# Reordering the first microseconds of a sparse attention and two-layer MoE kernel

## The chip, the cores and the metric

The kernel runs on one core of a Trainium2 chip. The metric is the device time of one execution in microseconds; lower is better. The kernel before has a median of 600.24 us over 3 runs (599.21 to 602.61).

## The reference

The reference computes a blocked attention and passes its result through two feed-forward layers. All tensors are fp32.

```python
# attention: batch 2, 8 heads, 768 positions, head size 64; block 32, window 16
k_sum = k.reshape(B, H, nb, block, D).max(axis=3)
v_sum = v.reshape(B, H, nb, block, D).mean(axis=3)
scores_l = scale * q @ k^T      # kept where |i - j| < 16, else -1e9
scores_s = scale * q . k_sum + log(block)
a = exp(scores_all - max);  a = a / (sum(a) + 1e-9)
x = a @ concat(v, v_sum)        # -> (1536, 512)
# layer 1
h = max(x @ w_in, 0);  x = (h * h) @ w_out       # 512 -> 2048 -> 512
# layer 2: P, Q polynomials of h with coefficients a, b
out = (P(h) / (Q(h) + 1e-6)) @ w_out2
```

## The kernel before

The work has two parts. The attention stage handles 24 groups. A pair (two heads of one batch entry, `n`, 8 of them) has three groups `G`; a group is four windows of 64 queries. Behind it come layer 1 and layer 2, with every fp32 product made of three products of rounded halves on TensorE.

A group goes through the engines in this order. TensorE computes its scores (`scores(G)`, L465 against the keys, L474 against the block maxima) into PSUM. VectorE adds the mask and takes the row minimum (`masked`, L886). ScalarE takes the exponentials with their row sums (`exps`, L679). VectorE guards and inverts the sums (L893, L898). GpSimd multiplies by the inverse (`normalise`, L354). TensorE transposes (`turn`, L499), ScalarE copies the transposes out of PSUM (L706, tile `probT`), and TensorE multiplies with the values (`output`, L515). The value window of a pair (`vwin`) holds 96 rows loaded from memory and 24 rows of block means. For the means TensorE runs `summary(n)` (L485), ScalarE copies (`copy_sums`, L685), TensorE runs `gather(n)` (L492), ScalarE copies (`copy_summary`, L691), and GpSimd spreads them into the window (`spread`, L339). The block maxima of the keys are a reduction on VectorE (`block_max`, L871).

The order of the work on each engine is written out by hand, with one list per engine and semaphores between them. TensorE runs ahead: scores of groups 0 to 2 before the loop, group 3 and 4 in its first turn, and then four groups ahead. Before the first scores it multiplies zeros (`keep_busy`, L554), `WARM` times 512 columns.

All loads are issued by SP in program order, but for two of pair 0 that ScalarE issues at its start: the middle third of the keys and the first third of the queries (semaphore `q_first[0]`, for which scores of group 0 wait). SP issues the other two thirds of the keys, the rest of the queries, the value window of pair 0 in two halves of 288 KB, and then keys, queries and window of the next pairs, 384 + 384 + 576 KB each. From pair 3 on the keys wait for the scores of an earlier pair, since three buffers go round. ScalarE's stream begins with nine semaphore increments that give first credits; the two transfers stand behind them. On ScalarE the exponentials of groups 0, 1 and 2 come before the loop, with the copies of the means between, and turn `G` of the loop copies the transposes of group `G` and then takes the exponentials of group `G + 3`. On GpSimd the normalisations of groups 0 and 1 come first, and then the spread of group 0.

Of the kernel before, what the change touches and what calls it, by code (L numbers as in the profile page):

```python
# [28 lines left out]
P = 128  # L29
B, H, S, D = 2, 8, 768, 64  # L30
BLOCK, BAND = 32, 16
# [8 lines left out]
GROUPS = PAIRS * B * GPB  # L40
# [20 lines left out]
P_RING = 4  # L61
# [3 lines left out]
XPAIRS = GROUPS // 2  # L65
KP = S + 2 * BAND
THIRD = S // GPB
WARM = 3
SPLIT_AT = {9: 0, 10: 1, 12: 2, 13: 3, 15: 4, 16: 5}
SUMMARY_AT = [0] + [GPB * n - 2 - (n > 2) for n in range(1, NB)]  # L70

# [11 lines left out]
def build(nc, qT, kT, vw, w1, w2, coef_a, coef_b, out):  # L83
# [43 lines left out]
    q, kraw, vwin = [], [], []  # L127
# [44 lines left out]
    k_first = [sem(f"k_first{i}") for i in range(GPB)]  # L172
# [4 lines left out]
    q_first = [sem(f"q_first{i}") for i in range(2)]  # L177
# [25 lines left out]
    norm_done = sem("norm_done")  # L203
# [36 lines left out]
    @block.sync  # L240
    def _(sp):
        def load_k(n):
            if n >= RING:
                sp.wait_ge(s_done, GPB * (n - RING + 1) + 1)
            sp.dma_start(kraw[n % RING][:, BAND:BAND + S], kT[n]).then_inc(k_in[n % RING], 16)

        def load_k_first(i):
            sp.dma_start(kraw[0][:, BAND + THIRD * i:BAND + THIRD * (i + 1)],
                         kT[0][:, THIRD * i:THIRD * (i + 1)]).then_inc(k_first[i], 16)

        def load_q(n):
            if n >= RING:
                sp.wait_ge(s_done, GPB * (n - RING + 1) + 2)
            sp.dma_start(q[n % RING][:, :], qT[n]).then_inc(q_in[n % RING], 16)

        def load_vwin(n):
            if n >= 2:
                sp.wait_ge(s_done, GPB * (n - RING + 2) - (n == 2))
            if n >= V_RING:
                sp.wait_ge(o_done, done(2, GPB * (n - V_RING + 1) - 1))  # L260
            for half in (slice(0, NW // 2), slice(NW // 2, NW)):
                sp.dma_start(vwin[n % V_RING][0:KW, half, :], vw[n][:, half, :]).then_inc(vw_in[n % V_RING], 16)

        def load_first(j):
            sp.dma_start(wraw[:, j:j + 1, :], w1[j:j + 1].rearrange("a p n -> p a n")).then_inc(w_first[j], 16)

        def load_weights(w, j, index, turn):
            if not (isinstance(turn, int) and turn == 0):
                sp.wait_ge(w_in[index], 16 * turn)
            sp.dma_start(wraw[:, bass.ds(j, 1), :], w[bass.ds(j, 1)].rearrange("a p n -> p a n")).then_inc(w_in[index], 16)  # L270

        load_k_first(0)
        load_k_first(2)
        sp.dma_start(q[0][:, THIRD:], qT[0][:, THIRD:]).then_inc(q_first[1], 16)
        load_vwin(0)
        for n in range(1, NB):
            load_k(n)
            load_q(n)
            if n >= NB - 1 - EARLY and n < NB - 1:
                load_first(n - NB + 1 + EARLY)  # L280
            load_vwin(n)
        sp.dma_start(ca[:, :], coef_a.partition_broadcast(P)).then_inc(coef_in, 16)
        sp.dma_start(braw[:, :], coef_b.partition_broadcast(P)).then_inc(coef_in, 16)
        for j in range(EARLY, FT // 2):
            if j < EARLY + 3:
                sp.wait_ge(s_done, GROUPS - 2 + j - EARLY)
            else:
                sp.wait_ge(o_done, done(2, GROUPS - 7 + j - EARLY))
            load_weights(w1, j, *landing(j))
        sp.wait_ge(o_done, done(2, GROUPS - 1))  # L290
        with sp.Fori(0, FT // 2 // LAND) as k:
            for i in range(LAND):
                load_weights(w1, LAND * k + FT // 2 + i, *landing(FT // 2 + i, k))
        with sp.Fori(0, FT // LAND) as k:
            for i in range(LAND):

                sp.wait_ge(b_done, done(2, (NCH - 1) * FT + LAND * k + i))
                load_weights(w2, LAND * k + i, *landing(FT + i, k))
        rows = out.rearrange("(n p) d -> n p d", p=P)
        with sp.Fori(0, NCH) as c:  # L300
            for t in range(ROWS):
                sp.wait_ge(o_copied, done(ROWS, ROWS * c + t))
                sp.dma_start(rows[bass.ds(ROWS * c + t, 1)].rearrange("a p d -> p a d"),
                             osb[:, t:t + 1, :]).then_inc(out_written[t], 16)
        for t in range(ROWS):
            sp.wait_ge(out_written[t], 16 * (NCH + 1))
# [3 lines left out]
    def _(pool):  # L310
# [30 lines left out]
        def spread(G):  # L341

            n, gi = divmod(G, GPB)
            if gi == 0:
                pool.wait_ge(vsum_copied, n + 1)
                if n >= V_RING:
                    pool.wait_ge(o_done, done(2, GPB * (n - V_RING + 1) - 1))
            pool.wait_ge(norm_done, min(G + 2, GROUPS))
            copy(vwin[n % V_RING][KW:COLS, GU * gi:GU * (gi + 1), :],
                 vsum[n % 2][KW:COLS, :].unsqueeze(1).to_broadcast([NBLK, GU, P])).then_inc(spread_done, 1)  # L350

        def normalise(G, r):
            pool.wait_ge(inv_done, G + 1)
            g.tensor_tensor(prob[r][:, :, :], prob[r][:, :, :],  # L354
                            inverse[r][:, :].unsqueeze(2).to_broadcast([P, GU, COLS]), ALU.mult).then_inc(norm_done, 1)
# [7 lines left out]
            pool.wait_ge(sem_hi, n + 1)  # L363
            g.tensor_tensor(wlo[index], wraw[index], whi[index].bitcast(F32), ALU.subtract).then_inc(sem_lo, 1)

        for G in range(2):
            normalise(G, G)
        spread(0)
        pool.wait_ge(spread_done, 1)

        def split_in(x):

# [64 lines left out]
    def _(pe):  # L437
# [5 lines left out]
        def scores(G):  # L443

            n, gi = divmod(G, GPB)
            r = n % RING
            if n == 0 and gi < 2:
                pe.wait_ge(q_first[gi], 16)
            if gi == 0:
                if n > 0:  # L450
                    pe.wait_ge(q_in[r], 16 * (n // RING + (r > 0)))
                if n == 0:
                    pe.wait_ge(edges, 1)
                    for part in range(GPB):
                        pe.wait_ge(k_first[part], 16)
                else:
                    pe.wait_ge(k_in[r], 16 * (n // RING + (r > 0)))
            pe.wait_ge(s_free, done(2, G - 2))

            for j in range(GU // 2):  # L460
                for e in range(2):
                    w = GU * gi + 2 * j + e
                    for h in range(2):
                        rows = slice(D * h, D * h + D)
                        mm(sps[G % 2][h][QW * e:QW * e + QW, j * COLS:j * COLS + KW], q[r][rows, QW * w:QW * w + QW],  # L465
                           kraw[r][rows, QW * w:QW * w + KW], start=True, stop=True)
            if gi == 0:
                pe.wait_ge(ksum_done, GPB * (n + 1))
            for j in range(GU // 2):
                for e in range(2):  # L470
                    w = GU * gi + 2 * j + e
                    for h in range(2):
                        rows = slice(D * h, D * h + D)
                        last = mm(sps[G % 2][h][QW * e:QW * e + QW, j * COLS + KW:(j + 1) * COLS],  # L474
                                  q[r][rows, QW * w:QW * w + QW], ksum[r][rows, :], start=True, stop=True)
            last.then_inc(s_done, 1)
# [82 lines left out]
        pe.wait_ge(consts, 4)  # L559
        scores(0)  # L560
        scores(1)
        pe.wait_ge(means_done, 1)
        summary(0)
        scores(2)
        pe.wait_ge(pick_ready, 4)
        keep_busy(2 * P)
        gather(0)
# [1 line left out]
        for G in range(GROUPS):  # L569
            turn(G, G % P_RING)  # L570
            ahead = 4 if G else 3
# [84 lines left out]
    @block.scalar  # L656
    def _(act):
        a = nc.scalar
        act.sem_inc(probT_done, 2)
        act.sem_inc(o_copied, ROWS)  # L660
        act.sem_inc(h_free, 2)
        act.sem_inc(y_free, KT)
        for t in range(ROWS):
            act.sem_inc(out_written[t], 16)

        act.dma_start(kraw[0][:, BAND + THIRD:BAND + 2 * THIRD], kT[0][:, THIRD:2 * THIRD]).then_inc(k_first[1], 16)
        act.dma_start(q[0][:, 0:THIRD], qT[0][:, 0:THIRD]).then_inc(q_first[0], 16)
        a.preload_act_table_set("natural_log_exp_and_others")
        act.wait_ge(consts, 3)
        act.wait_ge(means_clear, 1)  # L670
# [28 lines left out]
        copy_sums(0)  # L699
        exps(1, 1)  # L700
        copy_summary(0)
        exps(2, 2)
        for G in range(GROUPS):
            act.wait_ge(t_done, done(P_RING, G))
            act.wait_ge(o_done, done(2, G - 2))
            a.copy(probT[G % 2][:, :], tps[0:COLS, :]).then_inc(probT_done, 1)  # L706
            if G + 3 < GROUPS:
                exps(G + 3, (G + 3) % P_RING)
            if G == GROUPS - 2:
                relu(0, 0)  # L710
            for n in range(1, NB):
                if SUMMARY_AT[n] == G:
                    copy_sums(n)
                if SUMMARY_AT[n] + 1 == G:
                    copy_summary(n)
# [366 lines left out]
```

## Time and profile before

| | us |
|---|---|
| median of 3 runs | 600.24 |
| the profiled execution | 599.46 |
| its span in the profile | 597.6 |
| PE (TensorE) busy | 585.5 |
| DVE (VectorE) busy | 411.2 |
| ACT (ScalarE) busy | 290.0 |
| POOL (GpSimd) busy | 153.1 |

The span is what the profile's rows cover; the rest of the execution's time lies around it. PEld is TensorE's load of stationary operands, which overlaps its products. DVEq, ACTq and SPq are the instruction sequencers of the engines, which issue the transfers. The attention stage takes about the first 75 us.

### The profile page before, as it was taken

The page shows a single profiled execution, that of the slowest core. Times are in us where ns is not written, and L with a number is a line of the kernel's source. Part 1 is how long each engine was busy: PE and PEld are TensorE (multiplying, and loading weights), DVE is VectorE, ACT ScalarE, POOL GpSimd, SP SyncE. Part 2 cuts the span into 40 slices and gives each one's busy share as a digit, 9 for nine tenths or more (in the row PEclk, how much of TensorE's full clock was granted, in tenths as well). Part 3 has the DMA queues.
Part 4 walks back from the last instruction along what each step waited for, and adds up shares of the span by engine and source line. Part 5 has one row for each costly group of instructions (what it writes and reads, how often), then busy time and mean ns, then how long its engine had stood idle before and what let it go on. Part 6 is the DMA issues. An engine that isn't in the chain of part 4 may idle for free.

```text
span 597.6 us, 10616 instructions
## 1 busy us (share of the span) xinstructions
PE 585.5 (98%) x3770; PEld 479.4 (80%) x3770; DVE 411.2 (69%) x787; ACT 290.0 (49%) x613; POOL 153.1 (26%) x159
## 2 busy tenths in 40 slices
PE   7998999999999999999999999999999999999996
PEld 4777788888888888888888888888888888888884
DVE  5888796664433333456666788888888888888885
ACT  4888610111311101310111887777877767877775
POOL 4678810000120000300000355353242212231221
PEclk9999999999999999999999999999999999999999
DMA  8984570000000000032233200000100000100001
GB/s 254 261 242 109 168 281 1 0 1 0 2 0 0 0 0 0 0 107 83 94 105 106 70 1 1 0 0 1 71 0 0 0 0 0 71 0 1 0 1 70
DMA packets 11186, 31.42 MB, mean 53 GB/s; under 512 B 1552, under 2 KB 2064, under 8 KB 11152
## 3 DMA queue, kind: packets, MB, share of 16 engines
q1 hardware_dynamic: 10864, 30.68, 16.2%
q8 instruction: 24, 0.39, 0.3%
q10 hardware_dynamic: 288, 0.26, 0.1%
q14 instruction: 10, 0.08, 0.0%
HBM read 27.79 MB, written 3.15 MB: 52 GB/s over the span
## 4 chain that ended last, share of the span: by engine, by line
PE 50%; DVE 28%; issue 9%; ACT 7%; POOL 3%; DVEq 1%; ACTq 0%; POOLq 0%
PE bank L529 23%; PE bank L596 21%; DVE ratio L1024 6%; DVE numer L1006 6%; DVE ratio L1018 5%; DVE numer L1004 5%; DVE ratio L1013 5%; ACT hhi L764 5%; PE bank L515 2%; PE bank L499 1%; POOL prob L354 1%; ACT prob L679 1%; POOL vwin L339 1%; PE bank L465 1%; PE bank L554 1%
## 5 line engine op out<-in xcount | busy, mean ns | idle before, releaser
L529 PE MATMUL bank<-xhi,whi 128*128 (+1 forms) x384 | 149.9, 390 | 0.0
L529 PE MATMUL bank<-xhi,wlo 128*128 (+1 forms) x384 | 149.5, 389 | 0.0
L529 PE MATMUL bank<-xlo,whi 128*128 (+1 forms) x384 | 149.4, 389 | 0.0
L696 ACT ACTIVATE hsq<-bank 128x512 f32<-128x512 f32 x48 | 28.7, 598 | 213.3 <-PE bank L529 213.2
L407 POOL TENSOR_TENSOR denom<-denom,habs 128x512 f32<-128x512 f32 (+1 forms) x49 | 65.8, 1342 | 246.1 <-ACT denom L775 246.1
L529 PEld LDWEIGHTS bank<-xhi,whi 128*128 128x128 f32 x384 | 72.1, 188 | 15.0
L529 PEld LDWEIGHTS bank<-xhi,wlo 128*128 128x128 f32 x384 | 72.0, 188 | 15.0
L529 PEld LDWEIGHTS bank<-xlo,whi 128*128 128x128 f32 x384 | 72.1, 188 | 14.8
L613 PE MATMUL bank<-whi,hhi 128*128 128x512 f32 x192 | 74.8, 390 | 1.9 <-DVE hlo L1029 1.9
L1029 DVE TENSOR_TENSOR hlo<-ratio,hhi 128x512 fp32r<-128x512 f32 (+1 forms) x49 | 50.9, 1039 | 35.1 <-ACT hhi L764 35.1
L613 PE MATMUL bank<-wlo,hhi 128*128 128x512 f32 x192 | 74.7, 389 | 0.0
L613 PE MATMUL bank<-whi,hlo 128*128 128x512 f32 x192 | 74.7, 389 | 0.0
L596 PE MATMUL bank<-hhi,whi 128*128 128x512 f32 x192 | 74.7, 389 | 0.0
L596 PE MATMUL bank<-hlo,whi 128*128 128x512 f32 x192 | 74.7, 389 | 0.0
L596 PE MATMUL bank<-hhi,wlo 128*128 128x512 f32 x192 | 74.7, 389 | 0.0
L928 DVE TENSOR_TENSOR hsq<-hsq 128x512 f32<-128x512 f32 x48 | 34.0, 709 | 50.2 <-ACT hsq L696 50.2
L931 DVE TENSOR_SCALAR hhi<-hsq 128x512 fp32r<-128x512 f32 x48 | 21.4, 445 | 64.0 <-PE bank L596 63.8
L397 POOL TENSOR_TENSOR xlo<-xraw,xhi 128x512 fp32r<-128x512 f32 x12 | 19.2, 1624 | 165.1 <-ACT xraw L734 165.1
L772 ACT ACTIVATE habs<-bank 128x512 f32<-128x512 f32 x48 | 28.9, 602 | 52.7 <-PE bank L529 52.7
L613 PEld LDWEIGHTS bank<-whi,hhi 128*128 128x128 f32 x192 | 36.0, 188 | 10.0 <-issue 2.6
L613 PEld LDWEIGHTS bank<-whi,hlo 128*128 128x128 f32 x192 | 36.1, 188 | 7.6
L596 PEld LDWEIGHTS bank<-hhi,wlo 128*128 128x128 f32 x192 | 36.1, 188 | 7.5
(78 smaller groups left out, 890.5 us busy)
## 6 DMA issues: line engine op xcount, KB each, us to landing
wraw<-w SPq DMA_DIRECT2D x32, 512.0 KB, 3.4
vwin<-vw SPq DMA_DIRECT2D x16, 288.0 KB, 4.8
out<-osb SPq DMA_DIRECT2D x12, 256.0 KB, 2.1
kraw<-kT SPq DMA_DIRECT2D x7, 384.0 KB, 5.4
q<-qT SPq DMA_DIRECT2D x7, 384.0 KB, 4.5
kraw<-kT SPq DMA_DIRECT2D x2, 128.0 KB, 2.7
q<-qT SPq DMA_DIRECT2D x1, 256.0 KB, 4.6
kraw<-kT ACTq DMA_DIRECT2D x1, 128.0 KB, 3.3
```

Source lines behind the costliest of these rows:

```text
L407: g.tensor_tensor(denom[:, i, cols], denom[:, i, cols], habs[:, i, cols], ALU.mult).then_inc(q_done, 1)
L529: last = mm(hps[j % 2][:, :], W[a][:, j, kt * P:(kt + 1) * P], X[b][:, kt, bass.ds(CH * c, CH)], start=kt == 0 and i == 0, stop=kt == KT - ...
L596: last = mm(acc[dt][:, :], W[a][:, j, KT * P + dt * P:KT * P + (dt + 1) * P], HID[b][:, j % 2, :], start=j == 0 and i == 0, stop=j == FT - ...
L613: last = mm(acc[t][:, :], HID[a][:, j % 2, t * P:(t + 1) * P], W[b][:, j, KT * P:], start=j == 0 and i == 0, stop=j == FT - 1 and i == 2)
L764: a.copy(hhi[:, i, cols], ratio[:, cols]).then_inc(hi_done, 1)
L928: d.tensor_tensor(hsq[:, i, :], hsq[:, i, :], hsq[:, i, :], ALU.mult).then_inc(sq_done, 1)
L1004: d.tensor_tensor(numer[:, i, :], hps[i][:, :], numer[:, i, :], ALU.mult).then_inc(horner_done, 1)
L1006: d.scalar_tensor_tensor(numer[:, i, :], numer[:, i, :], ca[:, 1:2], hps[i][:, :], ALU.subtract, ALU.mult).then_inc(h_free, 1)
L1013: d.scalar_tensor_tensor(ratio[:, cols], denom[:, i, cols], one[:, 0:1], rcp0[bank][:, cols], ALU.add, ALU.mult).then_inc(t1_done, 1)
L1018: d.scalar_tensor_tensor(ratio[:, cols], ratio[:, cols], -2.0, rcp0[bank][:, cols], ALU.add, ALU.mult).then_inc(t2_done, 1)
L1024: d.scalar_tensor_tensor(ratio[:, cols], numer[:, i, cols], ca[:, 0:1], ratio[:, cols], ALU.subtract, ALU.mult).then_inc(ratio_done, 1)
L1029: d.tensor_tensor(hlo[:, i, cols], ratio[:, cols], hhi[:, i, cols].bitcast(F32), ALU.subtract).then_inc(g_ready, 1)
```

## The change

Seven edits, all in the first microseconds of the program:

```diff
-WARM = 3
+WARM = 2
@@ SP
         sp.dma_start(q[0][:, THIRD:], qT[0][:, THIRD:]).then_inc(q_first[1], 16)
+        sp.wait_ge(q_first[0], 16)
         load_vwin(0)
@@ GpSimd, in spread(G)
-            pool.wait_ge(norm_done, min(G + 2, GROUPS))
+            pool.wait_ge(norm_done, min(G + 2, GROUPS) if G else 1)
@@ GpSimd
-        for G in range(2):
-            normalise(G, G)
+        normalise(0, 0)
         spread(0)
         pool.wait_ge(spread_done, 1)
+        normalise(1, 1)
@@ TensorE
         scores(0)
         scores(1)
+        keep_busy(P)
+        scores(2)
         pe.wait_ge(means_done, 1)
         summary(0)
-        scores(2)
@@ ScalarE: the two dma_start move ahead of the nine sem_inc
+        act.dma_start(kraw[0][:, BAND + THIRD:BAND + 2 * THIRD], kT[0][:, THIRD:2 * THIRD]).then_inc(k_first[1], 16)
+        act.dma_start(q[0][:, 0:THIRD], qT[0][:, 0:THIRD]).then_inc(q_first[0], 16)
         act.sem_inc(probT_done, 2)
         ...
-        act.dma_start(kraw[0][:, BAND + THIRD:BAND + 2 * THIRD], kT[0][:, THIRD:2 * THIRD]).then_inc(k_first[1], 16)
-        act.dma_start(q[0][:, 0:THIRD], qT[0][:, 0:THIRD]).then_inc(q_first[0], 16)
@@ ScalarE
         exps(1, 1)
         copy_summary(0)
-        exps(2, 2)
         for G in range(GROUPS):
             act.wait_ge(t_done, done(P_RING, G))
             act.wait_ge(o_done, done(2, G - 2))
             a.copy(probT[G % 2][:, :], tps[0:COLS, :]).then_inc(probT_done, 1)
-            if G + 3 < GROUPS:
-                exps(G + 3, (G + 3) % P_RING)
+            for ahead in (2,) if G == 0 else (2, 3) if G == 1 else (3,):
+                if G + ahead < GROUPS:
+                    exps(G + ahead, (G + ahead) % P_RING)
```

With it, the copy of the first transposes precedes the exponentials of group 2, and the copy of the second transposes precedes those of group 3 and 4; from turn 2 on the order is as before. The spread of group 0 waits for normalisation 0 alone. SP issues the value window of pair 0, and all that follows, once the first third of the queries has landed.

## Rows read from the trace of the kernel before

**Rows 1.** The page's busy line, span and engines.
```profile
PE 585.5 (98%) x3770; PEld 479.4 (80%) x3770; DVE 411.2 (69%) x787; ACT 290.0 (49%) x613; POOL 153.1 (26%) x159
```

**Rows 2.** Stretches: from:to and length, then busy per engine, PEclk, DMA share, GB/s.
```profile
75.00:95.00 20.00, 20.00 (x89) 16.54 (x90) 18.38 (x27) 2.40 (x4) 2.12 (x2) 1.00 0.57 211
```

**Rows 3.** Chain that ended last, in order of time: start, duration, what.
```profile
1.81 4.59 PE bank L554 x6
...
6.64 0.54 PE bank L465 x14
...
13.83 0.59 ACT probT L706
...
14.47 0.69 PE bank L515 x16
...
32.99 0.05 ACT probT L706
...
38.16 0.99 POOL prob L354
...
57.75 0.63 POOL vwin L339
```

**Rows 4.** Line L554, two stretches: duration ns min/median/max, first to last start.
```profile
L554 PE MATMUL bank<-probT x2: 1007/1034/1061, 3.7 to 4.5; 120*128 120x512 f32 x2
...
L554 PE MATMUL bank<-probT x3: 592/593/1007, 4.5 to 5.8; 120*128 120x512 f32 x3
```

**Rows 5.** Timeline, the first issues of transfers: start, duration, engine, line.
```profile
0.82 0.87 SPq L248 DMA_DIRECT2D kraw<-kT  x2
1.35 0.39 ACTq L666 DMA_DIRECT2D kraw<-kT  x1
1.77 0.45 ACTq L667 DMA_DIRECT2D q<-qT  x1
2.21 0.90 SPq L262 DMA_DIRECT2D vwin<-vw  x2
```

**Rows 6.** Transfers issued at 1.77, 2.68 and 13.70: size, us to landing.
```profile
q<-qT ACTq DMA_DIRECT2D x1, 128.0 KB, 4.8
...
vwin<-vw SPq DMA_DIRECT2D x1, 288.0 KB, 5.8
...
kraw<-kT SPq DMA_DIRECT2D x1, 384.0 KB, 6.9
```

**Rows 7.** Stretches of 2 us; the last two columns are DMA share and GB/s.
```profile
2.00:4.00 2.00, 2.00 (x3) 0.97 (x4) 1.10 (x5) 1.66 (x4) 1.57 (x9) 1.00 0.81 225
4.00:6.00 2.00, 2.00 (x4) 0.55 (x3) 1.32 (x6) 0.00 (x0) 0.23 (x2) 1.00 1.11 332
6.00:8.00 2.00, 1.72 (x65) 1.25 (x64) 0.35 (x3) 0.00 (x0) 0.00 (x0) 1.00 0.97 237
...
18.00:20.00 2.00, 2.00 (x57) 1.70 (x54) 1.97 (x12) 1.95 (x10) 1.52 (x3) 1.00 1.06 288
```

**Rows 8.** Timeline of the front: start, duration, operation, [idle before <-releaser].
```profile
4.40 1.07 DVE L871 TENSOR_REDUCE ksum<-kraw 128x8 f32<-128x256 f32 x3
...
8.59 0.86 PE L485 MATMUL bank<-vwin,means 96*32 96x128 f32 x24 [0.62 <-issue]
...
10.11 0.24 ACT L685 COPY sums<-bank 128x128 f32<-128x128 f32 x1
...
13.54 0.62 POOL L339 TENSOR_SCALAR vwin<-vsum 24x512 f32<-24x512 f32 x1 [0.18 <-POOL prob L354]
```

**Rows 9.** Timeline of groups 4 to 6, 20 to 26 us.
```profile
20.62 0.42 DVE L871 TENSOR_REDUCE ksum<-kraw 128x8 f32<-128x256 f32 x1 [0.40 <-DMA kraw<-kT]
...
21.56 0.28 DVE L886 CUSTOM_DVE_ANT_0 prob<-bank,mask 128x120 f32<-128x120 f32 x1
...
22.59 0.40 ACT L679 ACTIVATE prob<-prob,lowest 128x120 f32<-128x120 f32 x1
...
24.11 0.56 ACT L706 COPY probT<-bank 120x512 f32<-120x512 f32 x1
...
25.43 0.90 PE L515 MATMUL bank<-probT,vwin 120*64 120x64 f32 x16
```

## The prediction
> **What bounds the kernel now.** I read the page's busy line first: TensorE is busy 98% of the span [rows 1]. The table of stretches shows where it isn't: from 75 us on TensorE has no hole (20.00 busy of 20.00), while the first 6.6 us hold only its warm-up passes [rows 2, 3]. No edit touches anything behind the attention stage, which ends near 75 us, so the change is worth exactly the shift of that stage's end. Then I followed the chain of waits in order of time [rows 3]. It is warm-up until 6.40, then scores of group 0 at 6.64, the masking on VectorE, three sets of exponentials on ScalarE (until 13.81), the copy of the first transposes at 13.83, and from 14.47 to 32.97 TensorE alone; after that a piece of ScalarE, and from 38.16 to 58.4 GpSimd without a hole, then TensorE to the end. A gain at the front counts only if it is still there at 33 us, when the chain leaves TensorE, and no transfer or engine in between has swallowed it.
>
> **The start: warm-up, ScalarE's transfers.** Scores of group 0 need the first third of q, ScalarE's second transfer. It was issued at 1.77 and landed 4.8 us later, at 6.57 [rows 5, 6]; the warm-up ended at 6.40. Both hold the 6.64, so both edits are needed. ScalarE runs nine semaphore increments first and issues at 1.35, where SP issues at 0.82 [rows 5]: moving the issues ahead gives at most 0.5 us. SP's wait keeps the two halves of the first value window (288 KB each) out of the way. Ahead of the wait 768 KB, 0.79 MB, are left; the stretches moved 0.45 MB by 4.0 us and then 332 GB/s [rows 7], so they have passed by 5.0, and with some lag to the semaphore q is there at about 5.3. Bounds: 4.8, and 6.1 if its 4.8 us stay as they are and only the issue moves.
> Each warm-up is two passes of 512 columns. The passes that start at 3.7 and before take 1061 ns, the fourth starts at 4.5 and takes 1007 ns, the last two 592 ns [rows 4]. The profile grants clock 1.00 in every stretch, yet I read 1061 against 592 ns as its two levels, 1.2 and 2.4 GHz. So two warm-ups end at 4.5 + 1.0 = 5.5, not at 6.40 less a third of 4.59 (4.9): the passes that go are the two fast ones, worth 0.9 us. Block maxima, also needed, are done at 5.47 [rows 8]. Scores of group 0 start at about 5.55 instead of 6.64: gain 1.1 us (0.5 with q at 6.1, 1.2 at best).
>
> **The value window.** Now it goes in at 5.35 and 5.8 instead of 2.21 and 2.68. From the moment q's bytes have passed (5.0) until the first bytes of the window flow (issue plus about 1.05, as 0.82 to the first traffic near 1.9, and inside the 2.1 us in which the first third of k landed) the engines have nothing to move: 1.4 us. Before, about 1.21 MB had moved by 6.4 [rows 7], now 0.79, and 0.42 MB at some 270 GB/s, between the 237 and 332 of those rows, are 1.55 us of lateness. The eight stretches from 4 to 20 us, of which three stand there, show the DMA engines full all the time (share 0.97 to 1.11), so nothing makes this up before 20 us. The window's second half landed 5.8 after 2.68, at 8.5 [rows 6]; I expect 9.2 (8.5 to 9.7). The first summary waited for it until 8.59 [rows 8]; it would now, behind scores of group 2, start at about 9.2 and end at 10.0, against 9.45. Its copy on ScalarE starts at 10.05 against 10.11 [rows 8], although the exponentials of group 0 are over at 9.1, not 10.2. So at this point the 1.1 us are gone: ScalarE stands and waits for the sums before it may do group 1's exponentials. Bounds for this copy: 9.4 (window at 8.5) to 10.6.
> Moving scores of group 2 ahead of the summary costs nothing, since it fills the wait, and the 128-column warm-up (about a quarter of a 512-column one, 0.3 us) lies there too.
>
> **Evicting ahead of the third exponentials.** Exponentials of group 1 end at 11.6 (before 11.88), the block mean's copy at 11.9, the transposes of group 0 end about 11.9 because their extra warm-up and gather start after the sums. The copy then runs 12.0 to 12.6 instead of 13.83 to 14.42 [rows 3]: the first output starts at about 13.5 instead of 14.47, behind scores of group 3, which wait for q and k of the second pair (one transfer later than before, 12.4). But the exponentials of group 2 start 0.5 us behind this copy, at 12.5, and end at 14.0 against 13.81, 0.2 us late (0.4 early to 0.9 late). Behind them wait, on VectorE in order, the guard and inverse of group 2, then the masking of groups 3 and 4, and GpSimd's normalisation 2. The edit takes 1.3 us off the first output and puts 0.2 us on this line; exponentials of group 3, before at 15.53, start at 15.5 to 16.2, after the second copy that now precedes them.
> **GpSimd.** Spread 0 waits for the mean's copy alone, so it runs 12.0 to 12.6 instead of 13.54 to 14.16 [rows 8]; without that the first output would wait for it. Normalisation 1 goes behind it: 12.7 to 13.7, before 12.37 to 13.36. Its transposes come after output 0 and scores of group 4 (14.7), so this 0.3 us is hidden; uncovered it would cost 0.3.
>
> **The third pair's keys.** The one wait on a transfer that the trace shows in this stage is VectorE's at 20.62, 0.40 us, for k of pair 3 [rows 9]. It was issued at 13.70, landed 6.9 later at 20.6 [rows 6], behind a full queue. The queue is late by 0 to 1.55 us now, so it lands at 20.6 to 22.2, say 21.6, although the compute ahead may be ready sooner. Nothing behind it on VectorE (masking 6, guard 5) can pass. What covers this: the masking ended four steps of 0.2 behind the reduction, at 21.85, and ScalarE began group 6's exponentials at 22.59, 0.7 us of slack; the copy at 24.11 was over at 24.67, and output 4 started at 25.43, 0.75 us more [rows 9]. Together 1.45 us of lateness do not reach TensorE's line. With k at 21.6, output 4 starts at 25.3 to 25.5; with k at 20.6 the exponentials start at 22.0, 0.6 us early, and output 4 with them.
> **Sum.** At output 4 the line stands between 0.6 us early and 0.2 us late. Taken: 0.2 us early, nearer the late end, because both the window and the keys of pair 3 come through the same late queue. Against the profiled execution, 599.46 (span 597.6 and 1.86 around it), that is 599.3; that execution lies 0.8 below the median 600.24 of the runs shown. From the median it gives 600.0. As the time of the new kernel's median I take 599.8, between the two.
>
> A page has a rule on the queues. The Trainium skill, "DMA: Bandwidth & Descriptors", section "Queues, rings and completion order", says that each DMA engine takes turns between the queues that have work for it. By that ScalarE's q, with 256 KB on its queue, would have been through when some 512 KB had moved in all, at about 4.3 us, whatever SP has queued behind its own q, and SP's wait would bring nothing. The trace disagrees: it landed at 6.57, when about 1.25 MB had moved. By the rule q would now be there at about 4.3 and the window enter the queue 1 us sooner, so the sum would be 0.6 early rather than 0.2.
>
> **Rivals.** *The front gain survives* (599.46 - 1.1 = 598.4; from the median 599.1). This needs the window by 8.6 and k of pair 3 by 20. For it: 332 GB/s were reached in one stretch, and the old window's landing lagged its bytes by 1.4 us, which an emptier queue might not. Against: the full shares until 20 us.
> *The queue's lateness goes through* (slower). SP's wait moves the window by 3.1 us, and everything behind it on SP by as much; if the queue recovers nothing, k of pair 3 lands at 23.7. The point from which it decides is 20.6 + 1.45 = 22.05; beyond it each microsecond is one on the line: +1.65, 601.1 from the profiled execution, 601.9 from the median. For it: the only transfer wait of the stage is on just this one. Against: k of pair 3 is issued by the compute (13.70), so the part of the lateness that the queue has by then worked off doesn't count.
> *The clock rises late.* TensorE's rise fell into the fourth pass, at about 5.2 us, with only that pass left of what now stays. Had it come later, scores of groups 0 and 1 (6.64 to 7.97, 1.33 us) would run at 1.2 GHz and take up to 1.33 us more, of which the path sees group 0's half, 0.7 (its part in the chain is 0.54 and 0.26): the gain of 1.1 becomes 0.4 and, with the window binding behind it, nothing else changes: 599.5, from the median 600.2. The trace bears it out little: the rise comes before the last of the four passes ends. The Trainium skill, "TensorE: Matmul & The Clock Gate", section "What's actually happening", says that where the rise falls varies from run to run; by that rule some executions have this 0.7 us and others not.
> *The change doesn't start earlier at all*: q at 6.1 or later because its 4.8 us are latency and not traffic. Scores start at 6.2, the window goes in at 6.15: the worst of both, 0.5 gained and 0.8 more lateness, +0.6: 600.1, from the median 600.8.
>
> **How the numbers follow.** Forecast 0.48, its own range 599.0 to 600.6; gain survives 0.22; lateness goes through 0.13; late clock 0.09; q stays late 0.08. The runs shown scatter from 599.21 to 602.61, which adds some 0.6 on either side. The range 598.3 to 601.8 leaves out the outer halves of the two far cases, less than 2 in 10. No case reaches 0.5% (3.0 us, about what a measurement here can tell from none), so only the scatter does: faster 0.05, same 0.91, slower 0.04.
>
> **What would show it.** In the new profile: four warm-up passes ending near 5.5; ScalarE's issues from 0.85; first scores 5.4 to 5.7; SP's value window issued at 5.0 to 5.6; TensorE idle ahead of the first summary, and ScalarE idle between exponentials 0 and the sums; first output 1 us early; VectorE waiting for k of pair 3 over 1 us. Wrong if the first summary starts before 8.6, or if the chain leaves TensorE near 33 us shifted by over 0.6 either way.

## The result: slower by 0.44%

| | us |
|---|---|
| before, median of 12 runs | 600.17 (598.28 to 603.93) |
| changed, median of 12 runs | 602.16 (599.88 to 605.16) |
| ratio | 1.0044, 95% interval 1.0027 to 1.0061 |
| the profiled execution of the changed kernel | 604.88, span 603.0 |

The forecast was 599.8 us with a range of 598.3 to 601.8. The measured time lies 0.4 us above that range, and the kernel is slower beyond its interval, so the prediction is wrong. In the profiled execution the span is 5.4 us longer (603.0 against 597.6). All of it has arisen by the point where the chain leaves TensorE.

The first view of the changed kernel is its chain in order of time (start, duration, what).

```profile
1.26 2.98 DMA q<-qT
...
5.58 7.57 DMA q<-qT
...
13.20 0.56 PE bank L466 x16
...
15.26 0.26 PE bank L500
15.51 1.57 issue
17.08 0.55 PE bank L500 x3
...
18.43 1.44 PE bank L486 x24
...
38.35 0.05 ACT probT L706
...
43.52 0.99 POOL prob L355
```

Against [rows 3]: the chain leaves TensorE at 38.35 instead of 32.99 and GpSimd's long stretch begins at 43.52 instead of 38.16, the same 5.36 us later. Three new things stand in it. The load of pair 1's queries takes 7.57 us and lands at 13.15. An "issue" of 1.57 us stands in the middle of the transposes of group 1, where TensorE waits for nothing that a semaphore shows. And the summary of the second pair (24 products) takes 1.44 us, where the chain of before has 0.79:

```profile
17.31 0.79 PE bank L485 x24
```

The timeline of the changed kernel shows the first microseconds (start, duration, operation, idle before and its releaser).

```profile
0.81 0.42 ACTq L661 DMA_DIRECT2D kraw<-kT  x1
...
1.26 0.46 ACTq L662 DMA_DIRECT2D q<-qT  x1
...
1.81 3.78 PE L555 MATMUL bank<-probT 120*128 120x512 f32 x4 [1.81 <-DVE probT L841]
...
4.26 0.81 SPq L262 DMA_DIRECT2D vwin<-vw  x2
...
5.52 0.92 PE L466 MATMUL bank<-kraw,q 64*64 64x96 f32 x16
...
8.90 0.86 PE L486 MATMUL bank<-vwin,means 96*32 96x128 f32 x24
...
9.84 0.27 ACT L686 COPY sums<-bank 128x128 f32<-128x128 f32 x1 [0.22 <-PE bank L486]
...
12.27 0.59 ACT L706 COPY probT<-bank 120x512 f32<-120x512 f32 x1 [0.36 <-PE bank L500]
...
13.20 0.56 PE L466 MATMUL bank<-kraw,q 64*64 64x96 f32 x16 [0.97 <-DMA q<-qT]
...
13.88 0.69 PE L516 MATMUL bank<-probT,vwin 120*64 120x64 f32 x16
...
17.08 0.55 PE L500 MATMUL bank<-ident,prob 128*120 128x128 f32 x3 [1.57 <-issue]
...
25.11 0.48 PE L516 MATMUL bank<-probT,vwin 120*64 120x64 f32 x4 [0.54 <-issue]
...
32.14 0.69 PE L516 MATMUL bank<-probT,vwin 120*64 120x64 f32 x16
```

The front itself does what the change intends: ScalarE issues 0.54 us earlier [rows 5], q is there at 4.24 instead of about 6.6, scores of group 0 start at 5.52, the first transposes are copied at 12.27 instead of 13.83 and output 0 starts 0.59 us earlier (13.88 against 14.47), although TensorE has by then waited 0.97 us for the queries of pair 1. Then TensorE stops for 1.57 us, and its clock falls. The stretches show that (the last three columns are PEclk, DMA share, GB/s).

```profile
14.00:16.00 2.00, 1.51 (x49) 1.22 (x49) 1.52 (x11) 0.37 (x2) 1.05 (x2) 1.00 1.04 259
16.00:18.00 2.00, 0.92 (x27) 0.75 (x28) 0.76 (x8) 0.34 (x1) 0.56 (x1) 1.00 1.05 227
18.00:20.00 2.00, 2.00 (x52) 1.50 (x44) 0.17 (x1) 2.00 (x11) 0.00 (x0) 0.51 1.06 244
...
28.00:30.00 2.00, 2.00 (x24) 1.55 (x26) 1.87 (x12) 0.80 (x6) 0.56 (x1) 0.50 0.49 144
30.00:32.00 2.00, 2.00 (x56) 1.84 (x56) 0.80 (x6) 2.00 (x9) 1.05 (x2) 0.58 0.78 314
32.00:34.00 2.00, 2.00 (x60) 1.61 (x52) 1.45 (x8) 0.89 (x4) 0.99 (x1) 1.00 0.92 269
```

TensorE works 0.92 of 2 us from 16 to 18; from about 18.0 to 31.7 (worked out from the shares 0.51 and 0.58 of the outer two stretches) it is granted 0.50, the 1.2 GHz level. Before, it was granted 1.00 in every such stretch.

How the 5.36 us come about can be added up. From the start of output 0 to the point where the chain leaves TensorE it takes 18.52 us before (14.47 to 32.99) and 24.47 now (13.88 to 38.35), 5.95 more. The pauses in it are 1.41 us before (0.2, 0.33 and 0.88) and 2.11 now (1.57 and 0.54), so they explain 0.70. The other 5.25 are products that take longer: an output of 16 products takes 1.05 us at 19.87 in the chain, where it took 0.61 at 18.11. Of this the earlier start gives back 0.59. The rows of before that this needs:

```profile
15.84 0.78 PE bank L499 x4
...
18.11 0.61 PE bank L515 x16
18.72 0.58 PE bank L499 x4
...
20.82 0.33 issue
...
30.93 0.88 issue
```

(The first pause, 0.2 us, is what four transposes take there beyond the 0.58 of the next group's.)

Each execution also lists its mean granted clock. Half clock for 12 us of 600 would be a mean of 0.99. I count an execution as one with a fall where the mean is 0.998 or less, and give the median span of the others beside it. (A mean of 0.999 can come from half clock in the last microsecond of the span, behind the last product, as in the profile of the kernel before with the loads of pair 2 held back.) "Before" is the kernel before, run beside the kernels of each of the three series of experiments below; for the series of the result itself its clocks are not on record.

| kernel | executions with a fall | span of the others, us |
|---|---|---|
| before (three series) | 7 of 35, 12 of 35, 2 of 29 | 597.1, 596.8, 597.4 |
| changed | 9 of 12 | 599.3 |

So the loss seems to have two parts: about 2 us also where the clock holds, and a fall in three of four executions instead of one in five. This compares across series, the first part rests on three executions, and how often before falls varies from series to series; the experiments below are therefore compared within their own series. The executions of before with a fall have a median span of 601.0, 599.9 and 599.7 us in the three series, 2 to 4 us above the others.

### The profile page after: what moved, and what is told of

It reads as the page before. It is cut to its first block, busy times and chain, and to the rows that moved or that the text cites. A ratio compares the mean times of both kernels' runs of the same rounds, so it can differ in the third digit from the quotient of the medians.

```text
span 603.0 us, 10616 instructions
## 1 busy us (share of the span) xinstructions
PE 590.8 (98%) x3770; PEld 484.1 (80%) x3770; DVE 411.2 (68%) x787; ACT 290.5 (48%) x613; POOL 153.4 (25%) x159
## 3 DMA queue, kind: packets, MB, share of 16 engines
q1 hardware_dynamic: 10864, 30.68, 15.6%
## 4 chain that ended last, share of the span: by engine, by line
PE 50%; DVE 28%; issue 9%; ACT 6%; POOL 3%; DMA 2%; DVEq 1%; SPq 0%; ACTq 0%; POOLq 0%
PE bank L530 23%; PE bank L598 21%; DVE ratio L1025 6%; DVE numer L1007 6%; DVE ratio L1019 5%; DVE numer L1005 5%; DVE ratio L1014 5%; ACT hhi L765 5%; DMA q<-qT 2%; PE bank L516 2%; PE bank L500 2%; POOL prob L355 1%; PE bank L466 1%; POOL vwin L340 1%; PE bank L486 1%
## 5 line engine op out<-in xcount | busy, mean ns | idle before, releaser
L530 PEld LDWEIGHTS bank<-xlo,whi 128*128 128x128 f32 x384 | 72.1, 188 | 14.7
L598 PEld LDWEIGHTS bank<-hlo,whi 128*128 128x128 f32 x192 | 36.0, 188 | 7.6
```

What stands on the lines that cost most here:

```text
L530: last = mm(hps[j % 2][:, :], W[a][:, j, kt * P:(kt + 1) * P], X[b][:, kt, bass.ds(CH * c, CH)], start=kt == 0 and i == 0, stop=kt == KT - ...
L598: last = mm(acc[dt][:, :], W[a][:, j, KT * P + dt * P:KT * P + (dt + 1) * P], HID[b][:, j % 2, :], start=j == 0 and i == 0, stop=j == FT - ...
```

## The experiments

Every kernel ran 12 times (one of them 6) beside the kernel before.

**First series.** The changed kernel without SP's wait:

```diff
-        sp.wait_ge(q_first[0], 16)
```


> The changed kernel without SP's wait for q_first[0]. Theory 1 (late queue, then clock): the wait puts the second pair's queries at 13.15 us instead of about 10.8, TensorE idles from 12.2 to 13.2 and again around 15.5 to 17, and the clock falls to 0.50 in many executions. Without the wait q of pair 1 lands by 11.5, no wait for it in front of scores of group 3, and the median is 599 to 600 (ratio to before 0.998 to 1.001). Theory 2 (one warm-up less): the granted clock is still lost in some executions, the median stays at 601.5 to 602.5. Theory 3 (the new order on TensorE's instruction stream moves its fetch stalls): a stall of over 1 us near 15.5 us is still there and so is the loss.

Measured: 601.51 us, ratio 1.0025 (1.0002 to 1.0047), a fall in 5 of 12, the others 597.9. That is above the 599 to 600 of theory 1. TensorE no longer waits for q of pair 1; a wait of 0.73 us stands elsewhere, ahead of scores of group 1, for the rest of the first pair's queries. But TensorE stands even longer at the same instruction:

```profile
5.40 0.56 PE L465 MATMUL bank<-kraw,q 64*64 64x96 f32 x16
...
6.88 0.56 PE L465 MATMUL bank<-kraw,q 64*64 64x96 f32 x16 [0.73 <-DMA q<-qT]
...
14.55 0.32 PE L499 MATMUL bank<-ident,prob 128*120 128x128 f32 x1
17.60 0.54 PE L499 MATMUL bank<-ident,prob 128*120 128x128 f32 x3 [2.73 <-issue]
```

Theory 1 alone does not hold: theory 3's stall is there. Whether taking the wait out gains anything can't be told from this run, since the intervals of 1.0025 and 1.0044 overlap; the run with the wait alone, below, tells more.

This run also shows what SP's wait was worth where it was meant to help. Scores of group 0 start at 5.40 without it and at 5.52 with it. ScalarE's q, issued at 1.26, landed like this without the wait (first row) and with it (second row, the changed kernel):

```profile
q<-qT ACTq DMA_DIRECT2D x1, 128.0 KB, 3.6
q<-qT ACTq DMA_DIRECT2D x1, 128.0 KB, 3.0
```

So without the wait q is there at 4.9 (at 4.3 in the second profile without the wait, below), and both are before the warm-up ends, at about 5.4. The wait brought the first scores nothing.

The changed kernel with `WARM = 3`:

> The changed kernel with WARM = 3. Theory 1: scores start at about 6.4 instead of 5.5, but SP's wait is still there and the value window and q of pair 1 land as late as in the changed kernel, so 601 to 602.5. Theory 2 (one warm-up less makes the clock fall): 599.5 to 600.5, granted clock 1.00 in all executions.

Measured: 602.59, ratio 1.0057 (1.0030 to 1.0084), a fall in 9 of 12, the others 598.9. The time is just above theory 1's range, and theory 2 falls. The stall moved, by exactly the two records that a third warm-up adds ahead of it, from behind the first of the transposes of group 1 to between records 15 and 16 of the products with the block maxima:

```profile
14.87 0.37 PE L475 MATMUL bank<-ksum,q 64*64 64x24 f32 x15
18.49 0.18 PE L475 MATMUL bank<-ksum,q 64*64 64x24 f32 x1 [3.25 <-issue]
```

It sits at a fixed place of the instruction stream, whatever the instruction there is: behind the 217th product record, counted from the first warm-up pass, in both kernels. The other profiles agree. I counted, from 14 to 90 us in all 14 of them, the pauses of over 0.12 us marked "issue" inside a run of equal products. Each stands behind record 217, 342, 468, 593, 718 or 968 (once 969), which are 125 or 126 records apart or a multiple of that; two profiles have none. With its weight load each product is two instructions, so a step is some 251 instructions, and 16 KB over 251 are about 65 bytes each (an estimate; the 16 KB are the packets below). So TensorE has run out of fetched instructions there.

The kernel before with SP's wait alone:

> The kernel before with SP's wait for q_first[0] alone. Theory 1: q_first lands some 0.3 later than in the changed kernel (ScalarE issues late), scores of group 0 stay at about 6.5, q of pair 1 lands after 13 us, and the whole loss and more appears: 601.5 to 603. Theory 2 and theory 3: within 0.5 us of before.

Measured: 603.90, ratio 1.0057 (1.0033 to 1.0081), a fall in 8 of 12, the others 599.9. The wait alone costs as much as all seven edits together, and lies above even the 601.5 to 603 of theory 1. Its profile has TensorE idle 2.04 us ahead of the first summary, whose window landed only at 9.45, and 2.54 us in the transposes of group 1:

```profile
9.54 0.86 PE L486 MATMUL bank<-vwin,means 96*32 96x128 f32 x24 [2.04 <-issue]
...
18.99 0.90 PE L500 MATMUL bank<-ident,prob 128*120 128x128 f32 x3 [2.54 <-issue]
```

The first of these two is marked "issue" as well, but it stands at the head of a group and ends with the landing of a transfer. "issue" alone does not say fetch.

The kernel before with `WARM = 2` alone:

> The kernel before with WARM = 2 alone. q_first lands at 6.57, so TensorE idles from 5.5 to 6.6 and nothing starts earlier. Theory 1: within 0.5 us of before. Theory 2: clock lost in some executions, 601 to 602.5.

Measured: 600.53, ratio 1.0012 (0.9989 to 1.0035), a fall in 6 of 12, the others 597.7. The time lies between the two expectations, and is unclear. There are more falls than in the 7 of 35 beside it, though not so many that chance is ruled out. In its profile the clock rises late: the products with the keys of groups 0 and 1 take 0.92 us each, where those of group 0 took 0.54 [rows 3]. In its profile, then, one warm-up less is not free; what it costs is less than the noise. The late rise does not come with it every time: the changed kernel without SP's wait has two warm-ups as well, and 0.56 at 5.40 above.

**Second series.** The changed kernel with ScalarE's old order:

```diff
         copy_summary(0)
+        exps(2, 2)
         for G in range(GROUPS):
```
(and in the loop only group G + 3, as before)

> The changed kernel with ScalarE's old order (exponentials of group 2 ahead of the copy of the first transposes), all else as changed, SP's wait too. Theory 1 (SP's wait starves TensorE): the loss stays, 601 to 603, since q of pair 1 still lands after 13 us and the instruction stall near 15 to 17 us is still there. Rival (the eviction ahead of the exponentials holds VectorE's masking of group 3 back): 599.5 to 600.5.

Measured: 602.46, ratio 1.0031 (1.0009 to 1.0053), a fall in 7 of 12, the others 598.7. ScalarE's order is not the cause. The stall at the first place is 0.20 us here, but there is one of 2.99 us from 20.3 us on, at the next place (behind record 342).

The loads of pair 2 held back, in the changed kernel without SP's wait:

```diff
+            elif n == 2:                      # load_k
+                sp.wait_ge(s_done, 3)
...
-                sp.wait_ge(s_done, GPB * (n - RING + 2) - (n == 2))
+                sp.wait_ge(s_done, 4 if n == 2 else GPB * (n - RING + 2))   # load_vwin
```

> The changed kernel without SP's wait, and with the loads of pair 2 held back: keys and queries until scores of group 2 are done, the value window until those of group 3. Theory 4 (TensorE's instruction fetch shares the DMA engines with the loads and is late because they are full from 4 to 20 us): the instruction packet starts and the stall near 15 us ends earlier, stall under 0.5 us, TensorE idles less, clock stays 1.00 in most executions, 597.5 to 599.5. Rival (the fetch takes its time whatever the loads do): the stall of 2 to 3 us stays, 601 to 602.

Measured: 599.87 (before 599.90 in this series), ratio 1.0009 (0.9985 to 1.0033), a fall in 1 of 12, the others 597.5. What theory 4 says of the stall holds: the 2.73 us are gone, and the transposes of group 1 come in one piece. The time is above its 597.5 to 599.5, and can't be told from that of the kernel without this edit (intervals 0.9985 to 1.0033 and 1.0002 to 1.0047, in two series). Three of the twelve executions took 603 to 604 us at a granted clock of 1.00; nothing here explains them.

```profile
15.58 0.65 PE L501 MATMUL bank<-ident,prob 128*120 128x128 f32 x4
16.92 0.56 PE L467 MATMUL bank<-kraw,q 64*64 64x96 f32 x16 [0.68 <-DVE lowest L888]
```

The profile has a queue of its own for instructions, one packet of 16 KB at a time. The packet ahead of this place starts at these times, and TensorE goes on 2.5 to 2.9 us later wherever it had to wait (the table has the runs below too):

| kernel | packet starts | TensorE reaches the place | goes on | stall |
|---|---|---|---|---|
| before | 13.6 | 15.9 | 16.1 | 0.2 |
| changed | 14.3 | 15.5 | 17.08 | 1.57 |
| changed, no SP wait | 14.8 | 14.9 | 17.60 | 2.73 |
| changed, WARM = 3 | 15.6 | 15.2 | 18.49 | 3.25 |
| changed, ScalarE's old order | 12.8 | 15.4 | 15.56 | 0.20 |
| before, SP wait alone | 16.2 | 16.5 | 18.99 | 2.54 |
| before, order edits alone | 13.4 | 15.3 | 16.03 | 0.74 |
| changed, pair 2 held back | 13.0 | 14.7 | 15.84 | 1.15 |
| changed, no SP wait, pair 2 held back | 12.3 | 15.7 | - | 0 |
| before, pair 2 held back (two profiles) | 12.3, 11.1 | 15.8, 16.7 | - | 0 |
| before, order edits, pair 2 held back | 11.0 | 16.0 | - | 0 |

The page of the changed kernel has the queue as a whole:

```profile
q8 instruction: 24, 0.39, 0.3%
```

The Trainium skill, "Runtime: NRT & Kernel Launch", section "Instruction fetch mechanics", says that an engine's instructions are refilled in 16 KiB blocks over a DMA queue of its own, and that the cost of crossing a block's boundary is mostly hidden. The trace agrees with the block (24 packets, 0.39 MB on that queue). In this stage the cost is not hidden: it is the 1.57 us above, and up to 3.25.

The same in the kernel before:

> The kernel before with the loads of pair 2 held back in the same way, nothing else changed. Theory 4: no stall at 16 us and a slightly earlier end, 598.5 to 600, fewer executions with a granted clock under 1.00. Rival: as before, 599.5 to 600.5, or slower by 0.5 if pair 2 then comes too late.

Measured: 599.14 against 599.90, ratio 0.9994 (0.9971 to 1.0017), a fall in 2 of 12. Packet at 12.3, no stall at 16 us. No gain that can be told.

The kernel before with the two order edits alone (ScalarE's copy ahead, spread 0 ahead of normalisation 1):

> The kernel before with the two order edits alone: first transposes copied ahead of the third exponentials, spread of group 0 ahead of the second normalisation. Theory: output of group 0 starts about 1.3 us earlier (13.1), TensorE then reaches the end of its fetched instructions at about 14.8 and stalls there until about 16, so the median is within 0.5 us of before, 599.3 to 600.5. Rival (the order edits carry a loss of their own): 600.5 to 602.

Measured: 599.63, ratio 1.0007 (0.9985 to 1.0028), a fall in 2 of 12. Output 0 starts at 13.65 instead of 14.47 (13.1 expected), and TensorE then stands at the place:

```profile
14.96 0.33 PE L499 MATMUL bank<-ident,prob 128*120 128x128 f32 x1
16.03 0.54 PE L499 MATMUL bank<-ident,prob 128*120 128x128 f32 x3 [0.74 <-issue]
```

The order edits neither lose nor gain anything that can be told.

**Third series.** The whole changed kernel, SP's wait too, with pair 2 held back:

> The whole changed kernel, SP's wait included, with the loads of pair 2 held back. If the instruction fetch behind a full queue is the larger part of the loss, the stall near 15 us shrinks to under 1 us and the median comes to 599.5 to 600.5; what is left against before is q of pair 1, still late, 0.5 to 1 us. If the late q of pair 1 alone takes the clock down, it stays at 601 to 602.5, with a granted clock under 1.00 in most executions.

Measured: 600.66 against 599.31, ratio 1.0019 (0.9999 to 1.0038), a fall in 4 of 12, the others 597.9. The stall is 1.15 us, not under 1. The time lies between the two expectations, nearer the first. That holding pair 2 back made the whole change cheaper is not shown: the intervals of 1.0019 and 1.0044 overlap. The stalls of 1.57 and 1.15 us also differ by less than the packet's start does between two executions of one kernel (12.3 and 11.1 in the table).

Order edits and pair 2 held back, in the kernel before:

> The kernel before with the two order edits and with the loads of pair 2 held back. If the order edits gained nothing only because TensorE then stood at its instruction fetch, they gain now: first output at about 13, no stall at 15 us, the end 0.5 to 1.3 us before that of the kernel before, 598.0 to 599.3. Rival: the line is swallowed elsewhere (the third exponentials, 0.2 us late by the prediction), 599 to 600, no better than with the loads held back alone.

Measured: 599.35 against 599.31, ratio 1.0000 (0.9987 to 1.0013), no fall in 12, and a spread of only 598.77 to 600.07. The time is the rival's: no better than with the loads held back alone. The stall is gone, and in its place scores of group 5 wait for VectorE's masking of group 3, which stands behind the guard of the third exponentials.

```profile
15.81 0.65 PE L501 MATMUL bank<-ident,prob 128*120 128x128 f32 x4
17.05 0.56 PE L467 MATMUL bank<-kraw,q 64*64 64x96 f32 x16 [0.59 <-DVE lowest L888]
```

In this profile the clock rose late and output 0 starts at 14.51, not at about 13, so it does not show what an earlier front would have met.

TensorE held idle on purpose, in the kernel before:

```diff
         for G in range(GROUPS):
+            if G == 1:
+                pe.wait_ge(vw_in[2], 32)
             turn(G, G % P_RING)
```

> The kernel before with TensorE held ahead of the transposes of group 1 until the value window of pair 2 has landed (19.3 us in the profile of before): an idle stretch of about 3 us from 16 us, with full instruction queue and unchanged loads. If such a stretch is what takes the clock down, the granted clock is under 1.00 in more than half of the executions and the median is 603 to 605 (3 us of idle and 1 to 3 for the clock). If the clock falls for another reason, it is under 1.00 in as few executions as before (a fifth to a third) and the median is at 602 to 603.

Measured (6 executions): 604.11, ratio 1.0098 (1.0065 to 1.0132), a fall in 6 of 6. The idle time ahead of the transposes is 1.56 us (16.58 to 18.14), not 3, since the window of pair 2 landed at 18.1 here and not at 19.3.

```profile
18.14 1.11 PE L499 MATMUL bank<-ident,prob 128*120 128x128 f32 x4 [1.56 <-DMA vwin<-vw]
```

```profile
16.00:18.00 2.00, 0.58 (x32) 0.47 (x28) 1.21 (x11) 1.62 (x8) 0.89 (x2) 0.95 0.87 216
18.00:20.00 2.00, 1.86 (x28) 1.52 (x30) 1.13 (x3) 0.71 (x2) 1.46 (x2) 0.50 0.54 171
...
22.00:24.00 2.00, 2.00 (x24) 1.54 (x28) 1.00 (x2) 0.23 (x1) 0.99 (x1) 0.50 0.76 247
24.00:26.00 2.00, 2.00 (x51) 1.70 (x52) 0.76 (x8) 1.97 (x9) 0.00 (x0) 0.84 0.03 8
```

A pause put in on purpose is followed by a fall of the clock in all six executions, with nothing else changed in the program. In the profile the clock falls at about 17.8 (granted 0.95 from 16 to 18), still inside the pause, and is back at about 24.6 (0.84 from 24 to 26). Of the 4.8 us lost, 1.6 are the pause; half clock for 6.8 us can add up to 3.4, half of it, if products take twice as long (an estimate).

Holding pair 2 back, once more:

> The kernel before with the loads of pair 2 held back, once more, since the first measurement (599.14 against 599.9) did not clear its interval. If the shallower queue helps: ratio 0.998 to 0.9995 again, and the clock under 1.00 in at most a sixth of the executions. If not: ratio at 1.000.

Measured: 599.52 against 599.31, ratio 1.0005 (0.9990 to 1.0020), a fall in 1 of 12. The time is that of before; the second "if" of the expectation holds.

## Why the prediction was wrong, step by step

The sum put the line at output 4 between 0.6 us early and 0.2 us late, with output 4 at 25.3 to 25.5. Output 4 started at 32.14, 6.7 us late. What failed is the term for the late queue: it had the harm at one place, VectorE's wait for the keys of pair 3, and at 0.2 us at most. The runs show it at TensorE: a wait for the queries of pair 1, a stall at its instruction fetch, and half clock behind both. The steps:

- *Warm-up and first scores* (5.55): right, 5.52, with the four warm-up passes over at 5.6 (5.5 forecast). But the clock's rise was later in this profile: the products with the keys of group 0 took 0.92 instead of some 0.55, and masking began at 7.06 (7.65 before), so 0.6 of the 1.1 us were left. The rival "clock rises late" described this.
- *ScalarE's q at 5.3, and "both edits are needed"*: q landed at 4.24, 3.0 us after its issue. The step failed in what it gave to SP's wait. Without the wait, and with ScalarE's earlier issue, q landed at 4.9 and 4.3 in two profiles, and scores of group 0 started at 5.40 and 5.35. The earlier issue alone was enough, and the edit that did the harm had no gain of its own. The prediction had this outcome in its paragraph on the turns between the queues, and set it aside.
- *The value window*: its second half took 3.6 us and was there at 8.2, not 9.2; the summary started at 8.90 and the sums' copy at 9.84 (10.05 forecast).
- *Eviction ahead of the third exponentials*: right in kind. Output 0 at 13.88 (13.5 forecast), and by itself without effect on the end (1.0007).
- *The queue's lateness*: here the prediction failed. It had q of pair 1 at 12.4 and looked for the harm at k of pair 3, behind 1.45 us of cover. q of pair 1 landed at 13.15, about 2.3 us later than before, and TensorE itself, not VectorE, stood in front of it for 0.97 us; the text names this wait and gives it no price. k of pair 3 landed at 22.4, later than the 21.6 taken, but the line was already late, and VectorE waits for no transfer at all. SP's wait alone costs 1.0057.
- *The missing term*: instruction fetch. The rows with its cause were in the chain of before: "issue" pauses of 0.33 and 0.88 us in the middle of a group of equal products, at 20.82 and 30.93, and the page has a queue named instruction. The sum took them as given. They are a deadline that an earlier front runs into: with the order edits alone output 0 was 0.8 us early, and TensorE then stood 0.74 us at this place.
- *The missing consequence*: the clock. The prediction weighs only when it rises, not that pauses at 12 to 18 us let it fall. It falls in 9 of 12 executions. In the profiled one the pauses behind output 0 add 0.70 us and the slower products 5.25, so the 5.36 us at the end of the chain's TensorE part are almost all clock. That execution is one of the slowest (604.88, median 602.16).
- *Chances*: slower by over 0.5% had 0.04; the measured 0.44% lies within "same", but above the range. The range was widened by 0.6 for the scatter of the runs before (602.61) without asking what made it. In the three series most of that scatter goes with falls of the clock, but not all: one execution of before has a span of 600.8 at a granted clock of 1.00. For the 602.61 no clock is on record.

That the loads of pair 2 make the packet late is borne out by four pairs of kernels, all the same way, with one or two profiles each: with them held back it starts at 12.3 instead of 14.8, at 13.0 instead of 14.3, at 12.3 and 11.1 instead of 13.6, and at 11.0 instead of 13.4, and the stall of 2.73 us is gone. That it is late because the DMA engines are full (share 1.0 there) is the likely reason, and is argued. Why it starts at 14.8 without SP's wait and at 13.6 in the kernel before, with nearly the same loads, stays open, as does why `WARM = 2` alone has 6 falls of 12. The stalls come from one profile of each kernel.

## What to carry to other kernels

A pause marked "issue" in the middle of a run of equal instructions was the instruction fetch here: see whether it stays at the same index when an instruction is added ahead, and keep the load queue shallow where the next block is due, before speeding up what comes ahead of it. A pause marked "issue" at the head of a group can be a transfer. Where a kernel's runs scatter, sort them by their granted clock first: here a change of 2 us was one in the work and one in how often TensorE's pauses cost it the clock. A wait on the queue that issues all loads moves every later load, and the first harm is at the next one due, not at the one that waited before. Where two edits aim at one wait, ask of each what it gives when the other is there.

## What the runs showed of the hardware

Six of the 14 profiles have a stretch at 1.2 GHz between 17 and 33 us. The longest pause of TensorE shortly before was 1.56, 1.57, 2.54, 2.73, 2.99 and 3.25 us; in the other eight no pause between 12 and 24 us is longer than 1.15. How long the low clock lasted does not follow the pause: some 13.7 us behind 1.57, 6.8 behind 1.56, 3.4 behind 3.25. And in the kernel before with SP's wait alone the 2.04 us idle up to 9.54 had no fall behind them (granted 1.00 until 18). An instruction packet of 16 KB, under a DMA share of 1.0, let TensorE go on 2.5 to 2.9 us after its start (eight stalls at the first place). ScalarE's transfer of 128 KB, issued at about 1.8 in the kernel before and its variants, landed after 3.6 to 4.8 us in seven profiles with the value window queued on SP, and after 3.6 in the one with the window held back. Issued at 1.26 it took 3.6 and 3.0 us with the window queued, and 3.0 to 3.4 with it held back.
